# Grouping the matmuls of a fused attention and MoE kernel into two runs a step, with one Sinkhorn normalization a step

## The reference

```python
def _attn_ref(q, k, v):                      # 4 x 8 heads, 576 positions, 64 wide
    scores = scale * np.matmul(q, k.transpose(0, 1, 3, 2))
    mask = (rel >= 0) & (rel < 64)
    attn = softmax(np.where(mask, scores, -1e9))
    return np.matmul(attn, v)

def _moe_ref(x, w_gate, w1, w2):             # N 2304, D 512, E 8, F 1024
    logits = x @ w_gate
    P = np.exp(logits - logits.max())
    for _ in range(8):
        P /= P.sum(1, keepdims=True) + 1e-09
        P /= P.sum(0, keepdims=True) + 1e-09
        P *= N / E
    for e in range(E):
        h = np.maximum(x @ w1[e], 0.0)
        out += P[:, e:e + 1] * (h @ w2[e])
```

## Time and profile before

| | |
|---|---|
| median of 3 runs | 1627.23 us (1627.09 to 1628.09) |
| the profiled execution | 1627.57 us, of which its span in the trace is 1625.8 us |
| PE busy | 98% of the span |
| POOL, DVE, ACT busy | 61%, 45%, 33% |
| mean granted TensorE clock | 0.995 of full |
| DMA | 74 GB/s over the span |

### The profile page before, as it was taken

The page is one execution under the profiler, slowest core; times in us unless marked ns, Lnnn a source line. Parts: engine busy times, 40 slices in busy tenths (PEclk is TensorE's granted clock), DMA queues, the critical chain, the costliest instruction groups (busy, mean ns, idle before and its releaser), DMA issues.

```text
span 1625.8 us, 24296 instructions
## 1 busy us (share of the span) xinstructions
PE 1595.2 (98%) x8880; PEld 1426.5 (88%) x8880; DVE 732.0 (45%) x1264; ACT 543.2 (33%) x774; POOL 998.5 (61%) x645
## 2 busy tenths in 40 slices
PE   7888999999999999999999999999999999999999
PEld 6877888888898888889888898888889888898888
DVE  5757634434434434434434344344344344344343
ACT  4742232332323333233232332334323333233331
POOL 5975555656556777565656656677565655656552
PEclk9999999999999999999999999999999999999999
DMA  7611212122121213212112121122211212122111
GB/s 216 180 54 52 74 56 78 52 77 75 54 77 52 77 52 117 78 52 78 65 64 77 52 77 63 66 77 91 78 62 68 78 52 77 57 72 77 52 65 39
DMA packets 34157, 120.41 MB, mean 74 GB/s; under 512 B 3904, under 2 KB 4160, under 8 KB 34112
## 3 DMA queue, kind: packets, MB, share of 16 engines
q1 hardware_dynamic: 34112, 119.80, 21.5%
HBM read 115.06 MB, written 4.72 MB: 74 GB/s over the span
## 4 chain that ended last, share of the span: by engine, by line
PE 94%; POOL 3%; DVE 2%; issue 1%; ACT 0%; POOLq 0%; DVEq 0%
PE ps L456 17%; PE ps L455 16%; PE ps L457 16%; PE ps L439 14%; PE ps L435 14%; PE ps L437 14%; POOL probs L756 1%; POOL sc L748 1%; PE ps L356 0%; PE ps L345 0%; PE ps L333 0%; DVE prob L1010 0%; DVE row_sum L985 0%; PE ps L502 0%; POOL t_raw L737 0%
## 5 line engine op out<-in xcount | busy, mean ns | idle before, releaser
L714 POOL TENSOR_TENSOR w_lo<-w_raw,w_hi 128x1792 fp32r<-128x1792 f32 (+2 forms) x98 | 391.0, 3990 | 529.5 <-ACT w_hi L548 529.4
L597 ACT ACTIVATE h_hi<-ps 128x384 fp32r<-128x384 f32 x384 | 189.0, 492 | 961.8 <-DVE ps L887 450.3
L456 PE MATMUL ps<-w_lo,h_hi 128*128 128x512 f32 x1152 | 457.0, 397 | 0.0
L457 PE MATMUL ps<-w_hi,h_lo 128*128 128x512 f32 x1152 | 456.6, 396 | 0.0
L455 PE MATMUL ps<-w_hi,h_hi 128*128 128x512 f32 x1152 | 455.3, 395 | 1.3 <-POOL w_lo L721 1.3
L439 PE MATMUL ps<-xv_hi,w_lo 128*128 128x384 f32 x1344 | 452.6, 337 | 0.0
L435 PE MATMUL ps<-xv_hi,w_hi 128*128 128x384 f32 x1344 | 450.8, 335 | 1.4 <-DVE logits L965 1.4
L437 PE MATMUL ps<-xv_lo,w_hi 128*128 128x384 f32 x1344 | 450.0, 335 | 0.0
L869 DVE SCALAR_TENSOR_TENSOR h_lo<-ps,h_hi 128x384 fp32r<-128x384 f32 x384 | 214.1, 558 | 361.6 <-ACT h_hi L597 360.9
L435 PEld LDWEIGHTS ps<-xv_hi,w_hi 128*128 128x128 f32 x1344 | 253.3, 188 | 31.4 <-DVE logits L965 1.5
L437 PEld LDWEIGHTS ps<-xv_lo,w_hi 128*128 128x128 f32 x1344 | 253.2, 188 | 29.1
(11 more groups left out here) (75 smaller groups left out, 948.1 us busy)
## 6 DMA issues: line engine op xcount, KB each, us to landing
w_raw<-w SPq DMA_DIRECT2D x192, 512.0 KB, 3.9
qk_buf<-qk SPq DMA_DIRECT2D x16, 576.0 KB, 5.5
v_win<-v SPq DMA_DIRECT2D x16, 288.0 KB, 4.3
...
```

The lines of the kernel that those rows point to most:

```text
L456: nc.tensor.matmul(ps_y[t], h_hi[slot][:, f, c], w2_lo[slot][:, f, :], start=False, stop=False)
L457: last = nc.tensor.matmul(ps_y[t], h_lo[slot][:, f, c], w2_hi[slot][:, f, :], start=False, stop=closes)
L597: nc.scalar.activation(h_hi[slot][:, f, half * HT:(half + 1) * HT], o, ACT.Relu)\
L714: last = nc.gpsimd.tensor_tensor(w1_lo[:, slot, c], w1_raw[:, slot, (lo + 1) * BLK:(hi + 1) * BLK], w1_hi[:, slot, c].bitcast(F32), ALU.su ...
```

## The change

1. **Order on PE.** The halves of the second product stand in two runs: 2 halves behind P7 and 10 behind P4 (`RUNS`), none behind P1, P6, P2, P5 and P3. So P3 of a step and P1, P6, P2, P7 of the next follow each other directly.
2. **Quarter 12.** `add_c12` writes its sum to `u4` in SBUF and no longer to the bank. ACT applies the relu to `u4` in place, waits for that, and copies `u4` to `h_hi`: two instructions in place of one. Its rest moves from DVE to POOL (`h12_rest`, 384 elements, the first work of POOL in the next step). P6 of the next step no longer waits for the rest but for the sum (`c_done`). DVE's next write to `u4` waits for POOL's rest.
3. **Sinkhorn.** One normalization in each of the steps 1 to 8, its column sums on PE behind P4. `row_sum`, `row_inv`, `col_sum` and `col_inv` are in PSUM, in the spare columns of the same bank. PE waits for `col_part` at P1 (at P4 in step 1). No wait for `logits_out` stands before step 1: it is at the last tile of its second product.
4. **What hangs on it.** The weights are final only in step 8, so expert 0 of the first block is taken unweighted (`tensor_copy`) in step 4, and ACT weighs its six tiles in step 8 (`weigh_first`, between `relu_21` and `relu_12`), ahead of the takes of expert 1. The diagonal of the maximum and the shift of the logits move to ACT (`max_spread_out`; the exponential takes the negative maximum as its bias). The six takes of a step stand otherwise in DVE's order: the first behind `add_u3`, four behind the rest of quarter 21, the last behind `add_c12`. More steps of the first block are unrolled.

```diff
+RUNS = [(0, 0), (0, 0), (0, 0), (0, 2), (2, 2), (2, 12), (12, 12)]
...
+        col_sum = [a[:, 0:E] for a in spread]
+        col_inv = [a[:, E:2 * E] for a in spread]
+        row_sum = [a[:, 2 * E:2 * E + NT] for a in spread]
+        row_inv = [a[:, 2 * E + NT:2 * E + 2 * NT] for a in spread]
...
                 elif k == P6:
-                    wait(pe, h_ready, n * 4)
+                    wait(pe, c_done, n * 3)
...
                 if t == TT // 2 and f == 0:
-                    pe.wait_ge(h_ready, n * 4 + 4)
+                    pe.wait_ge(h12_ready, n + 1)
...
-                for k, (lo, hi) in enumerate([(0, 2), (2, 4), (4, 6), (6, 8), (8, 10), (10, 11), (11, 12)]):
+                for k, (lo, hi) in enumerate(RUNS):
+                    if columns and k == P1:
+                        pe.wait_ge(col_part_ready, columns + 1)
                     if top and k == P7:
                         pe.wait_ge(max_all_ready, 1)
-                    if after_p6 is not None and k == P7:
-                        pe.wait_ge(chain, after_p6 * 8 + 5)
-                    if after_p7 is not None and k == P5:
-                        pe.wait_ge(chain, after_p7 * 8 + 5)
+                    if top and k == P4:
+                        pe.wait_ge(col_part_ready, 1)
                     multiply(s, first, n, slot, k)
                     if top and k == P6:
                         spread_max(1 - slot)
-                    if after_p6 is not None and k == P6:
-                        spread_columns(after_p6, 1 - slot)
-                    if after_p7 is not None and k == P7:
-                        pe.wait_ge(h_ready, n * 4 + 1)
-                        spread_columns(after_p7, slot)
-                    if after_p4 is not None and k == P4:
-                        spread_columns(after_p4, 1 - slot)
+                    if columns is not None and k == P4:
+                        spread_columns(columns, 1 - slot)
...
-            pe.wait_ge(logits_out, 1)
...
             def relu_12(n, slot):
                 act.wait_ge(c_done, n * 3 + 3)
-                relu(n, slot, bank[slot], 0, 1)
+                nc.scalar.activation(u4[:], u4[:], ACT.Relu).then_inc(c12_relu, 1)
+                act.wait_ge(c12_relu, n + 1)
+                nc.scalar.copy(h_hi[slot][:, 0, HT:TOKS], u4[:]).then_inc(h12_hi_ready, 1)
...
+            def max_spread_out():
+                act.wait_ge(max_part_out, 1)
+                nc.scalar.activation(max_diag[:], ident, ACT.Copy, scale=max_part[:, 0:1]).then_inc(max_part_ready, 1)
+
+            def weigh_first():
+
+                act.wait_ge(chain, SINKHORN * 8)
+                for t in range(TT):
+                    act.wait_ge(y_taken, t + 1)
+                    o = acc[:, 0, t * DM:(t + 1) * DM]
+                    at = place(0, t)
+                    nc.scalar.activation(o, o, ACT.Copy, scale=prob[:, at, 0:1]).then_inc(first_weighed, 1)
...
             relu_12(0, 0)
+            max_spread_out()
             w2_split(16, 0, 0)
...
+            def h12_rest(n, slot):
+
+                pool.wait_ge(h12_hi_ready, n + 1)
+                c = slice(HT, TOKS)
+                nc.gpsimd.tensor_tensor(h_lo[slot][:, 0, c], u4[:], h_hi[slot][:, 0, c].bitcast(F32), ALU.subtract)\
+                  .then_inc(h12_ready, 1)
...
             for n in (1, 2, 3):
+                h12_rest(n - 1, (n - 1) % 2)
                 window(n, n, landed(n + 2))
...
                 dve.wait_ge(prod_done, n * PRODUCTS + P5 + 1)
+                wait(dve, h12_ready, n)
                 nc.vector.tensor_tensor(u4[:], bank[slot], u2[:], ALU.add).then_inc(u4_done, 1)
...
                 dve.wait_ge(prod_done, n * PRODUCTS + P3 + 1)
-                nc.vector.tensor_tensor(bank[slot], bank[slot], u4[:], ALU.add).then_inc(c_done, 1)
+                nc.vector.tensor_tensor(u4[:], bank[slot], u4[:], ALU.add).then_inc(c_done, 1)
...
                 add_c22(n, slot)
+                if sinkhorn is not None:
+                    dve.wait_ge(col_sum_ready, sinkhorn + 1)
+                add_c21(n, slot)
                 rest(n, slot, bank[slot], 1, 1, 1)
...
                 rest(n, slot, bank[1 - slot], 1, 0, 2)
+                if sinkhorn is not None:
+                    columns(sinkhorn, 1 - slot)
+                    if not final:
+                        row_sums(sinkhorn + 1, 1 - slot)
+                        rows(sinkhorn + 1, 1 - slot)
+                some(0 if final else 1, 5)
                 add_c12(n, slot)
...
-                rest(n, slot, bank[slot], 0, 1, 3)
...
+                some(5, 6)
```

More of the change, by code:

```diff
@@ L523, in _ @@
                     n = s * PER_SB + j
-                    taken = None if n == 1 else n // FP * TT - 2 * TT
-                    if n == 1:
-                        window(s, False, n, j, taken, True, after_p4=0)
-                    elif n in (2, 3):
-                        window(s, False, n, j, taken, False, 3 * n - 5, 3 * n - 4, 3 * n - 3)
-                    elif n:
-                        window(s, j == 0, n, j, taken)
-                if s == 0:
-                    for j in range(FP):
-                        window(s, False, FP + j, j, TT - (2 * TT if j == 0 else TT), after_p6=None if j else 7)
-                with pe.Fori(1 if s else 2, E) as e:
+                    if n:
+                        window(s, j == 0, n, j, None if n == 1 else n // FP * TT - 2 * TT, n == 1,
+                               n - 1 if n <= SINKHORN else None)
+                if s == 0:
+                    for n in range(FP, 3 * FP):
+                        if n == SINKHORN + 1:
+                            pe.wait_ge(chain, SINKHORN * 8)
+                        window(s, False, n, n % FP, n // FP * TT - (2 * TT if n % FP == 0 else TT), False,
+                               n - 1 if n <= SINKHORN else None)
+                with pe.Fori(1 if s else 3, E) as e:
                     for j in range(FP):
@@ L642, in window @@
                 relu_21(n, slot)
+                if isinstance(n, int) and n == SINKHORN:
+                    weigh_first()
                 relu_12(n, slot)
@@ L681, in _ @@
                         window(n, landed(n), j)
-                with act.Fori(1, E - 1) as e:
+                if s == 0:
+                    for n in range(FP, 3 * FP):
+                        window(n, landed(n), n % FP)
+                with act.Fori(1 if s else 3, E - 1) as e:
                     for j in range(FP):
@@ L903, in take @@
                 weight = flat[:, at:at + 1] if isinstance(at, int) else flat[:, bass.ds(at, 1)]
-                if first:
+                if first and s == 0:
+                    nc.vector.tensor_copy(o, ps_y[t]).then_inc(y_taken, 1)
+                elif first:
                     nc.vector.tensor_scalar(o, ps_y[t], weight, None, ALU.mult).then_inc(y_taken, 1)
@@ L907, in take, with window @@
                     nc.vector.scalar_tensor_tensor(o, ps_y[t], weight, o, ALU.mult, ALU.add).then_inc(y_taken, 1)
[L909 removed]
+            def window(n, j, takes=None, top=False, sinkhorn=None):
                 slot = j % 2
[L914 removed]
+                final = sinkhorn == SINKHORN - 1
                 def some(lo, hi):
@@ L1038, in _ @@
             add_c12(0, 0)
[L1039 removed]
             find_max()
[L1042 to L1044 removed]
             for s in range(SB):
[L1046 to L1049 removed]
+                for j in range(FP):
+                    n = s * PER_SB + j
+                    if n:
+                        window(n, j, (s - 1, E - 1, False, n * TT - TT) if j == 0 else None, n == 1,
+                               n - 1 if n <= SINKHORN else None)
                 for j in range(FP):
                     n = s * PER_SB + FP + j
[L1052 to L1054 removed]
+                    window(n, j, (s, 0, True, n * TT - TT) if j == 0 else None, False,
+                           n - 1 if n <= SINKHORN else None)
+                if s == 0:
+                    for j in range(FP):
+                        n = 2 * FP + j
+                        window(n, j, (s, 1, False, n * TT - TT) if j == 0 else None, False,
+                               n - 1 if n <= SINKHORN else None)
+                with dve.Fori(2 if s else 3, E) as e:
                     for j in range(FP):
```

113 lines of the change are left out of this document (39 added, 74 removed).

## The result

The changed kernel takes **1645.56 us** (median of 4 runs, 1643.35 to 1645.91) where the kernel before takes 1627.32 (4 runs, 1627.09 to 1628.09): a ratio of 1.0108, 95% interval 1.0091 to 1.0126. It is slower, by 18.2 us by the medians and by 15.8 by the two profiled executions, where 15.6 were forecast (1643).

What follows compares the result with a forecast made beforehand. PE, busy 98% of the span, was taken to bound the kernel. The terms 17.3 + 4.4 + 3.2 - 10.3 + 1.0 = +15.6 on 1627.2 gave 1643 us, range 1628 to 1656.

Steps and rivals of the forecast that it cites:

- The stall in front of P2: Every step: PE waits for ACT's copy of P1, queued behind quarter 12; 0.33 us, uncertain from 0.22 to 0.40.
- The wait of ACT on itself: Between ACT's relu of quarter 12 and its copy to `h_hi`: taken as 0.03 us, uncertain up to 0.1.
- P6, for which 0.04 of room was worked out: P6 needs quarter 12's sum at 1.00, weight load due 1.04; if it doesn't fit, 0.1 us is lost.
- The longer run: Second product of each step: two runs of halves instead of seven take 8.24 us against 8.38, -0.14 a step.
- long runs bring nothing: Rival: the 0.2267 spacing belongs to the kernel's quiet end, so the -12.7 term falls away: 1656 us, 8%.
- A middle step: Steps 5 to 95: 15.66 - 0.14 + 0.33 = 15.85 us each, +17.3 over 91 steps.
- `x_split` in six steps: Ends of the first two blocks: `x_split` ahead of P1's copy delays P2 by 0.73 us, six times, +4.4.
- Steps 32 and 64: P5 waits 1.6 us because POOL's late work holds ACT's w1 split and the relu behind it; twice, +3.2.
- Sinkhorn (-10.3 and +1.0): Step 5 starts at 178.8 against 189.11 us, -10.3; steps 5 to 8 carry 0.25 each for a normalization, +1.0.
- The wait in front of P5 in step 1: In step 1, P5 comes at 117.3 where due near 113.2: a wait of 4.1 us, plus 3.0 for the clock.
- that rival: Rival: waits of 1.6 in steps 32 and 64 make the clock fall, +7 us, 1650; 12%.
- The price put on contention with the tiles in SBUF: Sinkhorn chains about 4.7 us longer, holding P1 by 1.4 seven times: +10; left out of the sum.

Runs made afterwards that it cites:

- p1_between: Changed kernel with ACT's copy of P1 between the relu and the `h_hi` copy of quarter 12, `x_split` behind them: 1614.45 us.
- seven_runs_dve: Changed kernel with the seven runs of halves of before, and DVE's rest of quarter 22 ahead of its addition to quarter 21 again: 1639.33 us.
- three_early: Changed kernel with three runs of halves (two in step 1), and relu of quarter 11 ahead of ACT's w1 split in steps 1, 2, 32, 64: 1601.66 us.
- tiles_sbuf: Changed kernel with `row_sum`, `row_inv`, `col_sum` and `col_inv` in SBUF again, schedule unchanged: 1649.83 us.

## Why the prediction was right

**The stall in front of P2, the largest term (0.33 in 95 steps).** Held, part by part. Counted from the last matmul of P3, predicted and measured: DVE's sum starts 0.38, 0.37; ACT's relu 0.97, 0.97; its copy to `h_hi` 1.53, 1.52; P1's copy 1.94, 1.94, for 0.48, 0.47. The pause is 0.21, and the late weight load 0.11: 0.32. The wait of ACT on itself, which no row of before showed, came out at the 0.03 taken for it (0.02 to 0.03 in every step). P6, for which 0.04 of room was worked out, doesn't wait. `p1_between` shows by removal that the cause is this queue on ACT: with only one of the two instructions of quarter 12 ahead of P1's copy the stall is zero.

**The longer run (-0.14).** Held: 0.227 in the middle of the kernel too, with all engines at work, which the rival "long runs bring nothing" denied. `seven_runs_dve`, `three_early` and `p1_between` give 15.66, 15.567 and 15.533 for seven, three and two runs without a stall: the whole is worth 0.127 a step. It follows that the trade was bad from the start: 0.13 gained for 0.32 paid, when a third run in front of P2 costs 0.034.

**A middle step.** 15.85 forecast, 15.86 measured, 15.92 to 15.95 in steps 16, 20 and 24 and 72 to 88 with j = 0; there P1's copy starts 0.05 to 0.08 later. ACT's loop begins a new pass in these steps. It does so in steps 40 to 56 of the second block too, and those take 15.85 to 15.88, so the pass alone doesn't explain it; the cause is open.

**`x_split` in six steps (+4.4).** Held. ACT's timeline of step 28, and P2 of that step in PE's:

```profile
545.25 0.83 ACT L564 CAST xv_hi<-x_raw 128x768 fp32r<-128x768 f32 x1
545.98 0.47 ACT L596 COPY p<-ps 128x384 f32<-128x384 f32 x1
```

```profile
546.50 0.44 PE L441 MATMUL ps<-xv_hi,w_hi 128*128 128x384 f32 x1 [0.78 <-ACT p L596]
```

The steps take 16.61: 0.75 more, six times 0.75 = 4.5.

**Steps 32 and 64 (+3.2).** Held: 17.46, 1.60 more each. The chain is the one worked out, over four engines. POOL's timeline, the rest of w2 and the last rest of the next block's x, behind which the four sums stand, then the end of the chain on POOL and DVE, then P5:

```profile
606.66 2.40 POOL L744 TENSOR_TENSOR w_lo<-w_raw,w_hi 128x1024 fp32r<-128x1024 f32 x1
609.01 1.85 POOL L772 TENSOR_TENSOR xv_lo<-x_raw,xv_hi 128x768 fp32r<-128x768 f32 x1
```

```profile
613.72 1.02 POOL L752 TENSOR_TENSOR h_lo<-u,h_hi 128x384 fp32r<-128x384 f32 x1
615.57 4.04 POOL L737 TENSOR_TENSOR w_lo<-w_raw,w_hi 128x1792 fp32r<-128x1792 f32 x1 [0.83 <-ACT w_hi L550]
```

```profile
615.91 0.56 DVE L904 SCALAR_TENSOR_TENSOR h_lo<-ps,h_hi 128x384 fp32r<-128x384 f32 x1 [3.86 <-ACT h_hi L599]
```

```profile
616.52 0.44 PE L441 MATMUL ps<-xv_hi,w_hi 128*128 128x384 f32 x1 [1.33 <-DVE h_lo L904]
```

**Sinkhorn (-10.3 and +1.0).** The wait in front of P5 in step 1 came as worked out, PE going on at 117.49 where 117.3 was forecast:

```profile
117.49 0.69 PE L441 MATMUL ps<-xv_hi,w_hi 128*128 128x384 f32 x1 [3.91 <-DVE h_lo L904]
```

Steps 2 to 8 hold no wait and cost 0.235 each (0.25). This term is the one that was off: P1 of step 5 starts at 177.47, not at 178.8, because the clock was at 1.2 GHz for 3.4 us only (117.1 to 120.5, the first 0.4 of them still in the wait) and cost 1.5 where I had taken 3.0; P1 of step 1 came at 106.99, 0.2 later than worked out. The window over most of step 1 and the start of 2 (columns: us, busy us of PE, PEld, DVE, ACT, POOL, then PEclk, DMA share, GB/s) has a PEclk of 0.91 where the earlier trace rows has 0.83:

```profile
110.00:130.00 20.00, 16.09 (x73) 14.00 (x74) 8.63 (x24) 4.31 (x7) 14.80 (x12) 0.91 0.29 106
```

Against the forecast the profiled execution thus has 1.3 us less here, 0.9 more for the middle steps (91 x 0.010) and 0.6 more for those with j = 0: 1643.35. That these cancel is luck. The median of the changed kernel lies another 2.2 above it, and no trace shows where its other executions spend that. A reading, not shown: their mean granted clock is 0.998 where the profiled one has 0.999, which one more stretch of 3.4 us at 1.2 GHz would give, and that costs 1.7; the traces of six of the other kernels have such a stretch between 86 and 94 us, that of the changed kernel none.

**The rivals.** The clock didn't fall in steps 32 and 64 of the changed kernel, behind waits of 1.6; it did in step 64 of `p1_between`, behind one of 2.0, and not in its step 32, behind the same 2.0. So that rival was real, and near. The price put on contention with the tiles in SBUF, seven times 1.4, was wrong: `tiles_sbuf` has it in one step, for 5.7 us of that step, 3.9 of waiting and 1.7 of clock. What the prediction left out is the instruction that sits beside the chain: only beside a long one of POOL does the delay grow past what the long run hides. The Trainium skill, page "SBUF — State Buffer", section "Who interferes with whom", says that a VectorE instruction with at most one SBUF input, outside the two-port modes, doesn't contend with GpSimd. The trace agrees: with the tiles in PSUM, `prob<-prob,ps` takes its usual 0.30 us beside a POOL instruction of 4.00.

**What the prediction didn't see** is that its sum isn't one of independent parts. Seven runs, with the changed order on DVE, cost 0.69 a step that the long run hides, and the Sinkhorn gain needs the long run too.
